# Token mixing on one core: angles three tiles ahead, turns four ahead, behind each step's products; the step's last sums placed at the head of VectorE's step

## What is computed

```python
x = windowed_attention(q, k, v)            # 8 heads of 64, window 128, 4 sink keys
theta = x @ w_theta                        # token mixing starts here
zr, zi = x * cos(theta), x * sin(theta)
y = einsum('ts,bsd->btd', w_tok_r, zr) + einsum('ts,bsd->btd', w_tok_i, zi)
u = x + y
m = u + maximum(u @ w_ch, 0)
gate = sigmoid(causal_conv(m, conv_w))     # 5 taps along the positions
out = (gate * (m @ w_val)) @ w_out
```

## Time and profile before

| what | value |
|---|---|
| device time, median of 3 runs | 643.74 us (642.96 to 644.14) |
| the profiled execution | 643.48 us |
| its span, first to last instruction | 641.7 us |
| TensorE busy in the span | 97% |
| VectorE, ScalarE, GpSimd busy | 64%, 46%, 42% |
| mean granted clock of TensorE | 0.998 of full |

### The profile page before, as it was taken

One profiled execution on the slowest core, in us unless ns is written; L12 is line 12 of the kernel. 1 busy time (PEld: TensorE's weight loads), 2 busy tenths in 40 slices (PEclk: granted clock), 3 DMA queues, 4 the chain that ended last, 5 costly groups with the idle time before them and its releaser, 6 DMA issues.

```text
span 641.7 us, 14247 instructions
## 1 busy us (share of the span) xinstructions
PE 624.0 (97%) x4016; PEld 539.1 (84%) x4016; DVE 412.5 (64%) x1026; ACT 293.1 (46%) x823; POOL 272.0 (42%) x340
## 2 busy tenths in 40 slices
PE   6999999999899999999999999999999999999995
PEld 4777777777788888888888888899899999999993
DVE  4888888887755366464643567869847647548550
ACT  5888988887333223232232334524334334334231
POOL 4787777782231213113122123455534534545420
PEclk9999999999999999999999999999999999999999
DMA  7777777765221243132511375321522021120011
GB/s 230 227 238 267 246 233 239 253 224 158 75 56 43 83 148 98 50 89 72 181 33 35 96 218 165 99 79 48 165 83 72 28 98 51 49 98 33 17 50 54
DMA packets 61337, 76.71 MB, mean 120 GB/s; under 512 B 4208, under 2 KB 41328, under 8 KB 61296
## 3 DMA queue, kind: packets, MB, share of 16 engines
q1 hardware_dynamic: 61296, 76.24, 37.0%
HBM read 51.06 MB, written 25.17 MB: 119 GB/s over the span
## 4 chain that ended last, share of the span: by engine, by line
PE 93%; DMA 2%; issue 2%; POOL 1%; DVE 1%; SPq 1%; ACT 0%; POOLq 0%; DVEq 0%
PE acc L1552 31%; PE ps_p L1601 19%; PE ps_th L1541 10%; PE ps_o L1641 10%; PE ps_s L542 7%; PE ps_y L598 7%; PE ps_t L565 3%; PE ps_t L570 2%; PE ps_o L612 2%; PE ps_x L1530 2%; DMA v_sb<-vP 1%; DMA q_sb<-qT 1%; DMA x_res<-xT_scratch 1%; PE ps_o L614 1%; POOL g_lo L1194 0%
## 5 line engine op out<-in xcount | busy, mean ns | idle before, releaser
L1162 POOL TENSOR_TENSOR z_lo<-z_raw,z_hi 128x512 fp32r<-128x512 f32 x47 | 61.4, 1327 | 206.0 <-ACT z_hi L1239 206.0
L1552 PE MATMUL acc<-w2h,z_hi 128*128 128x512 f32 (+1 forms) x384 | 131.2, 342 | 0.0
L1552 PE MATMUL acc<-w2l,z_hi 128*128 128x512 f32 (+1 forms) x384 | 129.3, 337 | 0.0
L1552 PE MATMUL acc<-w2h,z_lo 128*128 128x512 f32 (+1 forms) x384 | 129.3, 337 | 0.0
L349 ACT ACTIVATE probs<-masked,neg_max 128x132 f32<-128x132 f32 (+1 forms) x192 | 80.0, 421 | 22.9 <-DVE neg_max L431 19.6
L1552 PEld LDWEIGHTS acc<-w2h,z_lo 128*128 128x128 f32 x384 | 72.8, 190 | 8.0
L1552 PEld LDWEIGHTS acc<-w2l,z_hi 128*128 128x128 f32 x384 | 72.9, 190 | 7.8
L1552 PEld LDWEIGHTS acc<-w2h,z_hi 128*128 128x128 f32 x384 | 72.8, 190 | 7.9
L1355 DVE TENSOR_TENSOR xT_lo<-ps_x,xT_hi 128x512 fp32r<-128x512 f32 x24 | 16.6, 690 | 78.0 <-ACT xT_hi L1223 78.0
L1194 POOL TENSOR_TENSOR g_lo<-g_raw,g_hi 128x384 fp32r<-128x384 f32 x32 | 32.5, 1016 | 71.4 <-ACT g_hi L1295 71.4
L1465 DVE SCALAR_TENSOR_TENSOR ps_g<-m_raw,conv_w,ps_g 128x384 f32<-128x384 f32 x112 | 62.0, 616 | 0.2
(11 more groups left out here) (106 smaller groups left out, 1512.1 us busy)
## 6 DMA issues: line engine op xcount, KB each, us to landing
v_sb<-vP SPq DMA_DIRECT2D x16, 384.0 KB, 4.9
x_scratch<-x_sb SPq DMA_DIRECT2D x16, 384.0 KB, 2.7
x_nat<-x_scratch SPq DMA_DIRECT2D x24, 256.0 KB, 3.0
xT_scratch<-xT_raw SPq DMA_DIRECT2D x24, 256.0 KB, 2.2
x_res<-xT_scratch SPq DMA_DIRECT2D x24, 256.0 KB, 3.2
uT_scratch<-u_sb SPq DMA_DIRECT2D x24, 256.0 KB, 2.7
uT<-uT_scratch SPq DMA_DIRECT2D x8, 768.0 KB, 4.6
out<-o_sb SPq DMA_DIRECT2D x24, 256.0 KB, 2.0
```

The costliest lines, as they stand in the source:

```text
L1162: nc.gpsimd.tensor_tensor(z_lo[s % ZR][:, part, :], z_raw[:, part, :], z_hi[s % ZR][:, part, :].bitcast(F32), ALU.subtract).then_inc(z_lo_ ...
L1552: last = nc.tensor.matmul(bank, l, r, start=first and s == 0 and m == 0 and a == 0, stop=s == T - 1 and m == 1 and a == 2, skip_group_chec ...
```

## The change

Angles are now made three tiles ahead and turns four ahead, and in each step of TensorE they stand behind the products instead of ahead of them. For this the opening makes one more turn, one more angle and one more chain; theta of tile 1 of batch 0 is written into `acc[1]`, which the first products touch only at their second block, so it needs no free `ps_th`. VectorE's `add_x` calls move from the end of `token_body` to the head of step 5. SP's `store_xT`, GpSimd's and ScalarE's chains move by one tile in the same way, and `load_x` of tile 5 moves from the end of the body into step 5. The number of products is unchanged. The core of the diff (left out: the same in the path for other window sizes, which does not run here, the loops of GpSimd, and renamings):

```diff
--- before.py
+++ after.py
@@ -257,6 +257,7 @@
             mix.store_xT(0, 1)
             store_pair(PAIRS - 1, B - 1, 3, 1)
             mix.store_xT(0, 2)
+            mix.store_xT(0, 3)
 
             for s in range(2):
                 sp.wait_ge(x_out[s], 16 * PAIRS // 2)
@@ -404,12 +406,16 @@
             evac_sinks(PAIRS - 1)
             mix.xT(0, 1)
             mix.sine_table()
+            mix.xT(0, 2)
+            mix.sine(0, 0)
             evac_y(PAIRS - 1, 2)
-            mix.xT(0, 2)
-            mix.sines(0, 0)
+            mix.cosine(0, 0)
             mix.z_parts(0, 0)
+            mix.xT(0, 3)
             mix.sines(0, 1)
             mix.z_parts(0, 1)
+            mix.sines(0, 2)
+            mix.z_parts(0, 2)
             mix.run()
 
         @block.vector
@@ -514,12 +520,16 @@
             mix.turns_out(0, 0)
             mix.angle(0, 0)
             mix.xT(0, 2)
+            mix.z_parts(0, 0)
             normalise(PAIRS - 1, 1, IT - 1, False)
+            mix.cosine_lo(0, 0)
             mix.turns_out(0, 1)
-            mix.z_parts(0, 0)
-            mix.cosine_lo(0, 0)
             mix.angle(0, 1)
+            mix.xT(0, 3)
             mix.z_parts(0, 1)
+            mix.turns_out(0, 2)
+            mix.angle(0, 2)
+            mix.z_parts(0, 2)
             mix.run()
 
         @block.tensor
@@ -651,11 +661,13 @@
             pe.wait_ge(maxed, SCORES * PAIRS)
             mix.turn(0, 1)
             mix.theta(0, 0)
+            mix.turn(0, 2)
+            mix.theta(0, 1)
             pv(PAIRS - 1, 1, 2, IT)
             turn_y(PAIRS - 1, 1, 1)
             turn_y(PAIRS - 1, 1, 2)
-            mix.turn(0, 2)
-            mix.theta(0, 1)
+            mix.theta(0, 2)
+            mix.turn(0, 3)
 
             pe.wait_ge(normed, 2 * PAIRS)
             mix.run()
@@ -948,6 +961,15 @@
         ps_x = bank("ps_x", [P, CB, P])
         ps_th = bank("ps_th", [P, C])
         acc = [bank(f"acc{t}", [P, C]) for t in range(T)]
+
+        def angle_bank(b, s):
+
+
+            return acc[1] if first_angle(b, s) == 1 else ps_th
+
+        def first_angle(b, s):
+            return s if isinstance(b, int) and b == 0 and s < 3 else None
+
 
     with ExitStack() as channels_banks:
         def banks(name, count):
@@ -1106,13 +1128,15 @@
             for s in range(T):
                 if s > 0 and not last:
                     load_x(b + 1, s - 1)
+                if s == T - 1 and not last:
+                    load_x(b + 1, T - 1)
                 if last and s < len(W3_STEP):
                     for j in W3_STEP[s]:
                         load_w3(j)
-                if s < T - 3:
-                    store_xT(b, s + 3)
+                if s < T - 4:
+                    store_xT(b, s + 4)
                 elif not last:
-                    store_xT(b + 1, s + 3 - T)
+                    store_xT(b + 1, s + 4 - T)
                 if s == T - 2:
                     for j in range(RR):
                         load_res(b, j)
@@ -1124,9 +1148,6 @@
                 sp.dma_start(bank_of(uT_scr, b, j), two_halves(u_sb[j % RR], j)).then_inc(u_out[j % RR], 16)
                 if j < T - RR:
                     load_res(b, j + RR)
-            if not last:
-                load_x(b + 1, T - 1)
-
         def channel_body(b, last):
             for c in range(2):
                 if not last:
@@ -1251,14 +1279,14 @@
 
         def token_body(b, last):
             for s in range(T):
+                if s < T - 4:
+                    xT(b, s + 4)
+                elif not last:
+                    xT(b + 1, s + 4 - T)
                 if s < T - 3:
-                    xT(b, s + 3)
+                    chain(b, s + 3)
                 elif not last:
-                    xT(b + 1, s + 3 - T)
-                if s < T - 2:
-                    chain(b, s + 2)
-                elif not last:
-                    chain(b + 1, s + 2 - T)
+                    chain(b + 1, s + 3 - T)
                 if last and s < len(W3_STEP):
                     for j in W3_STEP[s]:
                         split_w3(j)
@@ -1359,12 +1389,13 @@
 
             n = T * b + s
             dve.wait_ge(theta_done, n + 1)
-            nc.vector.tensor_scalar(k_big[:], ps_th[:], 1.0 / (2 * PI), ROUND, ALU.mult,
+            bank = angle_bank(b, s)
+            nc.vector.tensor_scalar(k_big[:], bank[:], 1.0 / (2 * PI), ROUND, ALU.mult,
                                     ALU.add).then_inc(k_big_done, 1)
             dve.wait_ge(k_big_done, n + 1)
             nc.vector.tensor_scalar(k_int[:], k_big[:], -ROUND, None, ALU.add).then_inc(k_int_done, 1)
             dve.wait_ge(k_int_done, n + 1)
-            nc.vector.scalar_tensor_tensor(out=r_part[:], in0=k_int[:], scalar=-TWO_PI_HI, in1=ps_th[:],
+            nc.vector.scalar_tensor_tensor(out=r_part[:], in0=k_int[:], scalar=-TWO_PI_HI, in1=bank[:],
                                            op0=ALU.mult, op1=ALU.add).then_inc(r_part_done, 1)
 
         def angle(b, s):
@@ -1422,25 +1453,27 @@
 
         def token_body(b, last):
             for s in range(T):
+
+                if s == T - 1:
+                    if last:
+                        dve.wait_ge(conv_in, 16)
+                        dve.wait_ge(halo_zero, 1)
+                        relu_conv(0, 0)
+                    for j in range(T):
+                        if last and j < CB:
+                            gated(0, 0, j)
+                        add_x(b, j)
+                if s < T - 4:
+                    xT(b, s + 4)
+                elif not last:
+                    xT(b + 1, s + 4 - T)
                 if s < T - 3:
-                    xT(b, s + 3)
+                    chain(b, s + 3)
                 elif not last:
-                    xT(b + 1, s + 3 - T)
-                if s < T - 2:
-                    chain(b, s + 2)
-                elif not last:
-                    chain(b + 1, s + 2 - T)
+                    chain(b + 1, s + 3 - T)
                 if last and s < len(W3_STEP):
                     for j in W3_STEP[s]:
                         split_w3(j)
-            if last:
-                dve.wait_ge(conv_in, 16)
-                dve.wait_ge(halo_zero, 1)
-                relu_conv(0, 0)
-            for j in range(T):
-                if last and j < CB:
-                    gated(0, 0, j)
-                add_x(b, j)
 
         def relu_add(b, c, k):
             n = 2 * b + c
@@ -1533,12 +1566,13 @@
         def theta(b, s):
             n = T * b + s
             pe.wait_ge(xT_lo_done, n + 1)
-            wait_count(pe, r_part_done, n)
+            wait_count(pe, r_part_done, n if first_angle(b, s) is None else n - 1)
+            bank = angle_bank(b, s)
             for k in range(CB):
                 x = (xT_hi[s % XR][:, k, :], xT_lo[s % XR][:, k, :])
                 cols = slice(2 * T * S + k * C, 2 * T * S + (k + 1) * C)
                 for a, (l, r) in enumerate(split_passes(x, (w2h[:, cols], w2l[:, cols]))):
-                    last = nc.tensor.matmul(ps_th[:], l, r, start=k == 0 and a == 0,
+                    last = nc.tensor.matmul(bank[:], l, r, start=k == 0 and a == 0,
                                             stop=k == CB - 1 and a == 2)
             last.then_inc(theta_done, 1)
 
@@ -1559,6 +1593,9 @@
             for j in range(T):
                 if s == 0:
                     pe.wait_ge(u_done, T * b + j + 1)
+                    if j == 1:
+
+                        pe.wait_ge(r_part_done, T * b + 2)
                 if j < CB:
                     last = block_of(s, j, acc[j][:], slice(0, C), True)
                 else:
@@ -1573,17 +1610,17 @@
 
         def token_body(b, last):
             for s in range(T):
-                if s < T - 2:
-                    theta(b, s + 2)
-                elif not last:
-                    theta(b + 1, s + 2 - T)
-                if s < T - 3:
-                    turn(b, s + 3)
-                elif not last:
-                    turn(b + 1, s + 3 - T)
                 if last and s == T - 1:
                     first_channels()
                 tokens(b, s)
+                if s < T - 3:
+                    theta(b, s + 3)
+                elif not last:
+                    theta(b + 1, s + 3 - T)
+                if s < T - 4:
+                    turn(b, s + 4)
+                elif not last:
+                    turn(b + 1, s + 4 - T)
 
         def first_channels():
```

More of the change, by code:

```diff
@@ L57 @@
 PoolMix = namedtuple("PoolMix", "constants chain run")
-ScalarMix = namedtuple("ScalarMix", "begin sine_table xT sines z_parts run")
+ScalarMix = namedtuple("ScalarMix", "begin sine_table xT sine cosine sines z_parts run")
 VectorMix = namedtuple("VectorMix", "begin xT turns_out angle z_parts cosine_lo run")
@@ L333, in _ @@
             mix.chain(0, 1)
+            mix.chain(0, 2)
             mix.run()
@@ L923, in mixing @@
         conv_w = own("conv_w", [P, CB, TAPS], SMALL_AT + 32)
```

(20 more changed lines are left out.)

## The result

The changed kernel takes 654.0 us (median of 4 runs, 652.8 to 654.6) against 643.9 us (4 runs, 643.0 to 644.1) for the kernel before on the same chip: a ratio of 1.0164 with a 95% interval of 1.0148 to 1.018. It is slower, near the 652.7 us that were forecast. The profiled execution took 654.6 us with a span of 652.9 us.

What follows compares the result with a forecast made beforehand. TensorE, busy 624.0 of 641.7 us, was taken as the bound, so any new wait is paid in full. 643.48 - 2.0 (opening) + 11.1 (three boundaries) = 652.6, stated as 652.7 us; range 648 to 656.

Steps and rivals of the forecast that it cites:

- The opening: Before the first token product: theta(2) no longer waits for VectorE to read theta(1); gain 2.0 us, bounds 0 to 2.0.
- The loops: Loop bodies of TensorE, VectorE, ScalarE and GpSimd: sequences mostly only relabelled, costing and bringing nothing.
- SP's queue: Batch boundaries: tile 3's turn store, held for ScalarE's copy, delays u_sb stores and late reloads; theta(3) 3.9 us later at the first.
- The size: Loss at the three batch boundaries: 3.9 + 4.1 + 3.1 = 11.1 us, bounds 5.4 to 12.9.
- landing - 0.8: Loss per batch boundary: third late reload's time from issue to the sixth sum, less 0.8 us.
- 8.26 us of the formula: First batch boundary, kernel before: time from ScalarE's copy at 235.58 to theta(3) at 243.84, subtracted in the loss formula.
- The rival of quiet landings: Batch boundaries: reloads land in 2.6 to 3.3 us; loss 5.4 to 7.5, time 647 to 649.5; chance 0.15.
- Last batch: Eight weight splits behind the last angle, 2.7 us more, fit in VectorE's idle time; the 1.1 us m_raw wait stays.
- The sum: Whole kernel: 643.48 - 2.0 + 11.1 = 652.6 us for the profiled execution; 652.7 forecast as median.

Runs made afterwards that it cites:

- SP's queue undone: Changed kernel with SP's queue alone put back to the order of the kernel before: 640.5 us against 643.0 for the kernel before, ratio 0.9965.
- the queue alone: Kernel before with only SP's queue order taken from the changed kernel: 657.7 us, ratio 1.0222 to the kernel before.
- the one store: Changed kernel with the turn store of the next batch's tile 3 moved behind all six u_sb stores: 640.6 us against 642.9 before, 0.9963.
- the other execution: Second profiled execution, from running the unaltered changed kernel once more: 654.4 us against 642.9 before, ratio 1.0178; no fall of the clock.
- the transfer last: Changed kernel with SP's wait for tile 3's turn kept ahead of the u_sb stores, its transfer behind all six: 651.4 us against 643.8 before, 1.0121.
- behind the first reload: Changed kernel with the next batch's tile 3 turn store behind the first late reload: 648.9 us against 643.0 before, 1.0094.
- behind the second: Changed kernel with the next batch's tile 3 turn store behind the second late reload: 641.3 us against 642.9 before, 0.9971.
- the angle early: Changed kernel with VectorE's turns_out and angle of tile 2 ahead of the fourth sum: 651.6 us against 643.0 before, 1.012.
- The run with one bank: Changed kernel with SP's queue as before and theta of tile 1 in ps_th, not acc[1]: 649.4 us against 642.9 before, 1.0094.

## Why the prediction was right, step by step

**The opening.** Forecast 2.0, measured 2.23. The missing 0.25 is the restart: the theta group behind the wait had taken 3.03 us in the earlier trace rows, and one without a wait takes 2.8. `z_lo` started at 161.10, and VectorE had read `acc[1]` by 163.9, some 0.3 us ahead of block 1 at 164.18, where 0.2 was forecast.

**The loops.** Forecast nothing, and it is nothing: with SP's queue undone every step lasts 11.56 us.

**SP's queue.** The mechanism is shown from both sides, by the queue undone, by the queue alone, and by the one store. The pieces came as costed: 0.82 us from copy to store (0.82), 0.59 to the next issue (0.6), 2.93 to the third reload (2.9), 3.22 from the sixth sum to theta (3.15).

**The size.** Forecast 11.1, measured 14.4 in one execution and 13.8 in the other: the boundaries were priced 3.3 us too low, and of that a shorter attention part in the profiled execution hid 1.0 us by chance. Three things were off, all in the step "landing - 0.8".

- The landings were taken from the same boundaries before. The third reload took 4.98, 4.73 and 4.77 us where the prediction had 4.67, 4.86 and 3.88: 1.1 us more, nearly all of it at the third boundary. The 3.88 is the shortest of the eighteen landings with five transfers ahead that the traces hold (mean 4.7); to carry one boundary's own landing over was the weak point. In the other execution it took 5.07, 5.54 and 4.80.
- The restart was left out: 0.24 us wherever theta waits, 0.5 to 0.7 us in all. The 8.26 us of the formula end at 243.84, where the chain's piece begins, and the first matmul of theta(3) had started at 243.67, so from the copy on it is 8.09. The matmuls' own starts close the sum without a fitted term: from the copy's start to theta(3) it is now 12.55 us, 4.46 more, and the first boundary lost 4.45.
- The clock was left out: at the second boundary 5.74 us were lost where 4.73 - 0.8 + 0.25 = 4.2 answers to its landing: 1.5 us more.

With the restart the formula is landing - 0.55. It fits the five boundaries of the changed kernel without a fall to 0.05 us. Each transfer that no longer follows the wait takes its issue time off: landing - 1.14 with the transfer last (0.6 for the turn store), landing - 1.69 behind the first reload (1.15 for a store and a reload), landing - 2.83 behind the second (1.15 again). All nine boundaries of these three kernels fit to 0.05 us. The kernel with SP's new queue alone is off by up to 0.14. Only the landing itself has to be measured.

**The rival of quiet landings** fell. The fit in the Trainium skill's "DMA: Bandwidth & Descriptors", section "Anatomy of one DMA", is for GpSimd's path, and gives an estimate of 2.6 us for 256 KB; the trace has 4.98 for the third reload, behind six other transfers of that size in 3.5 us, and 3.13 behind two. Its other sentence, that the issuing sequencer waits and not the DMA engines, agrees with the run in which the wait alone cost 10.6 us.

**Last batch.** Eight splits stand behind the last angle and VectorE still idles 2.99 us before the `m_raw` at 438.49:

```profile
426.14 7.33 DVE L1441 TENSOR_TENSOR w_lo<-x_nat,w_hi 128x512 fp32r<-128x512 f32 x6 [1.21 <-ACT w_hi L1278]
433.65 1.86 DVE L1441 TENSOR_TENSOR w_lo<-x_nat,w_hi 128x512 fp32r<-128x512 f32 x2 [0.17 <-ACT w_hi L1278]
438.49 0.56 DVE L1482 SCALAR_TENSOR_TENSOR m_raw<-ps_p,uT 128x384 f32<-128x384 f32 x1 [2.99 <-PE ps_p L1638]
```

TensorE's wait for an `m_raw` further on stayed, 1.0 us against 1.1.

**The sum** of 652.6 for the profiled execution compares with its 654.6: 3.3 more at the boundaries, 0.23 less for the opening, and 0.98 less for an attention part that happened to be shorter.

## What to carry to other kernels

When an order is moved by one step, read each DMA queue as an instruction stream of its own, and ask of each issue what it waits for and which loads stand behind it: here one store, held for a copy of a tile that TensorE turns late, stopped reloads, and these stopped TensorE, 4.6 to 4.8 us on average at each of three boundaries. Moving that line alone turned 1.6% slower into 0.4% faster. Price a held queue by its last link, with the landing of a burst and not of a quiet transfer. And add to each new wait of TensorE its restart, and a possible fall of the clock.

## What the hardware showed that was not expected

- **The clock falls behind short stalls, in some executions.** In the changed kernel the granted clock went to 0.50 for 6.8 us behind a wait of 1.76 us. In its other trace waits of 1.73 and 1.83 us at the same boundary left it at full speed. Behind the opening's 1.97 us it stayed in the kernel before and fell in the one with SP's new queue alone. At the boundaries and the opening these traces hold 14 places with a wait of 1.6 to 2.0 us, and at five of them the clock fell (one in the changed kernel, two with SP's new queue alone, two with the angle early). The run with one bank isn't counted; there it fell during a wait of 4.3 us. Behind waits of 0.7 to 1.2 us (the wait alone at SP) and of 0.3 to 1.0 us (the store behind the first reload) it did not. A fall cost 1.0 to 1.6 us at four of the five, and about 0.1 us at the second boundary with SP's new queue alone, where the next wait took it in. What decides between two executions with like waits is open.
- **A wait costs 0.25 us more than the idle time shown.** Twelve matmuls of a theta group take 2.99 to 3.03 us behind a wait and 2.75 to 2.8 without, counted from the end of the group ahead; 0.17 us of it is that the first of them no longer overlaps that group. The first boundary agrees: waits of 1.73, 1.28 and 0.66 us are 3.67 together, and 4.45 us were lost.
- **The same 256 KB reload lands in 2.6 to 5.5 us.** It took 2.6 to 2.9 when the queue is quiet. The third late reload, to the start of its sum, took 3.1 to 3.2 behind two transfers sent just before, 4.4 to 4.5 behind four, 3.9 to 5.5 behind five (eighteen boundaries, the kernel before among them, mean 4.7) and 4.5 to 5.5 behind six (twelve, mean 4.9). So a few against many makes a difference, but five against six can't be told apart boundary by boundary. The count ahead isn't all either: in the changed kernel the second late reload, with only four ahead, landed in 4.6 to 5.4 us.
